# Two expert products replaced by products with the slot matrices in a routed mixture kernel on one Trainium2 core

## The chip, the cores and the metric

The kernel runs on one core of one Trainium2 chip. The metric is the device time of one execution in microseconds (us). The kernel before took 572.39 us, the median of three runs (568.43, 572.39 and 573.89 us).

## The reference, cut to what matters

Three stages follow each other. A decaying linear attention over 4 batches, 8 heads, 768 positions and head size 64 gives 3072 tokens `x` of 512 numbers. A mixture of experts sends each token to one of 8 experts. A second mixture ("slots") forms 32 weighted sums over all tokens, puts each through one of 8 further experts, and hands them back to all tokens.

```
logits = x @ w_gate;  e_idx = argmax(logits);  gate_w = softmax(logits)[e_idx]
eom = sigmoid(x @ w_output_gate)
h = relu(x[mask] @ w1[e])                    # 512 -> 1024, the tokens of expert e
y[mask] = gate_w * eom[mask, e] * (h @ w2[e])        # 1024 -> 512
# the slots, with y as their input
logits = y @ phi                             # 512 -> 32
d = softmax(logits, over the 3072 tokens);  slot_input = d.T @ y     # 32 x 512
slot_out[e] = relu(slot_input[e] @ v1[e]) @ v2[e]    # 4 slots for each of 8 experts
out = softmax(logits, over the 32 slots) @ slot_out
```

## The kernel before, in words

Five programs, one for each engine and one for the DMA queue of SyncE (SP), run in written order and meet at semaphores. There is no planner: the order of the lines is the schedule.

**Attention.** 24 steps of 128 tokens. TensorE (PE) forms scores, outputs and states in plain fp32. Each step also computes the gate logits and stores the finished rows to DRAM. SP loads q, k and v three steps ahead, expert 0's `w1` in between (`load_w1`, in four pieces), and after the last step's loads expert 0's `w2` (`load_w2`).

**Routing.** After the last step VectorE (DVE) finds each token's expert and its rank there. PE multiplies small bf16 matrices (L1256 to L1265) that turn ranks into lists of rows. POOL then gathers the rows of `x` by these lists (`gather_x`).

**Expert chunks.** `for i in range(MAIN)` at L1386 runs 8 chunks, one for each expert, with 432 token places in 4 groups of 108. A chunk does this:
- `x_turn` transposes the gathered rows on PE. ScalarE (`x_high`) and DVE (`x_low`) split the result into two fp32r halves.
- `w1_high`, `w1_low`, `w2_high` and `w2_low` split the weights in the same way, in place, in pieces of 128x1024.
- `h_tile` (8 tiles) and `y_tile` (4 tiles) are the products, 96 fp32r matmuls of 432 columns each per chunk, since `three_pass` multiplies high by high, low by high and high by low. `h_high` and `h_low` keep both halves of `relu(h)`; `y_keep` keeps `y` transposed.
- The slots' share of chunk `i-1` is woven between the h tiles of chunk `i`: `logit_parts` (y times phi, four matmuls side by side in four groups of 32 output partitions), `logits` (the sum of the four parts), `y_turn` (y back to rows), `logits_turn`, `p_turn`, and `acc_part` (p^T times y). On DVE belong to it `logits`, `slot_max`, `max_keep`, `slot_weights` and `accumulate`, on ScalarE `slot_exp`, on POOL `scatter_logits` and `gather_g`. It is a running softmax: `acc` and `ssum` are rescaled by `alpha` in each chunk.

A plain fp32 matmul stands in the trace as two instructions, a transpose or an fp32r matmul as one.

SP loads the next expert's `w1` when all h tiles of a chunk are done (four pieces of 512 KB), then one of the first four `v1` matrices (2 MB), and the next `w2` when all y tiles are done.

**Tail.** `combine_part(MAIN - 1)` does the slots' share of the last chunk by itself. `slot_stage` transposes the slot inputs (L1467), multiplies them with the eight `v1` (L1474), and the result with `v2` in halves (`second_product`), and writes the output in 12 groups (`out_group`). SP loads what is left of `v1` and `v2` there, as buffers come free.

An extra loop for experts with more than 432 tokens exists behind `If(n > MAIN)`; it did not run in this execution.

Of the kernel before, what the change touches and what calls it, by code (L numbers as in the profile page):

```python
# [21 lines left out]
F32 = mybir.dt.float32  # L22
# [3 lines left out]
ALU = mybir.AluOpType  # L26
# [93 lines left out]
def program(nc, qk_h, kv_h, wg_h, phi_h, w1_h, w2_h, v1_h, v2_h, const_h, yscale_h, out_h):  # L120
# [6 lines left out]
    with ExitStack() as ctx:  # L127
# [24 lines left out]
        w2_hi = put("w2_hi", [UNIT], F32R, at=unit(2))  # L152
        w2_raw = put("w2_raw", [UNIT], at=unit(3))
        w2_lo = put("w2_lo", [UNIT], F32R, at=unit(3))
        v_unit = put("v_units", [8, UNIT])
# [16 lines left out]
        acc = put("acc", [P])  # L172
# [8 lines left out]
        hTh = put("hT_hi", [FT, TC], F32R, at=b)  # L181
        hTl = put("hT_lo", [FT, TC], F32R, at=b)
        c_area = b[0]
        yT = put("yT", [KT, TC], at=b)
        yrow = put("y_rows", [NS, D], at=b)
# [8 lines left out]
        a = unit(4)  # L194
# [11 lines left out]
        assert a[0] <= unit(7)[0]  # L206
# [28 lines left out]
        r = [c_area]  # L235
# [9 lines left out]
        r = unit(7)  # L245
        rows = put("rows_hot", [T, SUB], BF16, at=r)
        tcols = put("tile_cols", [T, 3, TW], BF16, at=r)
        assert r[0] <= unit(8)[0]
# [23 lines left out]
        d = [c_area]  # L272
        rs = put("ssum_inv", [1], at=d)
        slotx = put("slot_in", [P], at=d)
# [23 lines left out]
        e = [h_area]  # L298
        v7 = put("v7", [UNIT], at=e)
        hTm = put("hT_masked", [FT, NE, SLOTS], at=e)  # L300
        assert e[0] <= c_area
# [3 lines left out]
        e = [h_area]  # L305
        cT = put("cT", [T, P], F32R, at=e)
        e = unit(3)
# [23 lines left out]
        s_w2 = [sem(f"s_w2_raw{i}") for i in range(NP)]  # L331
# [26 lines left out]
        s_hi1, s_hi2 = sem("s_w1_hi"), sem("s_w2_hi")  # L358
        s_lo1, s_lo2 = sem("s_w1_lo"), sem("s_w2_lo")
# [5 lines left out]
        s_H, s_hh, s_hl = sem("s_h_product"), sem("s_hT_hi"), sem("s_hT_lo")  # L365
        s_Y, s_yT = sem("s_y_product_b"), sem("s_yT")
        s_c1, s_lraw, s_c2, s_lc = sem("s_logit_parts"), sem("s_lraw"), sem("s_logits"), sem("s_lcur")
        s_c3 = sem("s_logits_turned")
        s_yr, s_yk = sem("s_y_turned"), sem("s_y_rows")
# [3 lines left out]
        s_c5, s_acc = sem("s_acc_product"), sem("s_acc")  # L373
# [10 lines left out]
        w1_v = w1_h.rearrange("e (k p) f -> e p k f", p=P)  # L384
        w2_v = w2_h.rearrange("e (k p) m -> e p k m", p=P)
        v1_v = v1_h.rearrange("e (k p) f -> e p k f", p=P)


        V_AT = [v_unit[:, n, :] for n in (4, 5, 6, 7, 0, 1)] + [v6[:, :], v7[:, :]]
        Q_AT = [v_unit[:, n, :].rearrange("p (f h m) -> p h f m", h=2, m=D // 2)[:, half] for half in range(2) for n in (2, 3)]  # L390
        Q_AT += [v_unit[:, n, :].rearrange("p (h f m) -> p h f m", h=2, m=D // 2)[:, half] for n in (4, 5, 6, 7, 0, 1) for half in range(2)]
        OUT_BANKS = ((0, 1), (6, 7))

        OUT = (0, 1, 4)
        Y_BANK = (2, 3, 6, 2)
        X_BANK = (5, 6, 7, 2)
# [29 lines left out]
        def _(sp):  # L426
# [20 lines left out]
            def load_w1(e_, p):  # L447
                sp.dma_start(piece_of(w1_raw, p), w1_v[e_][:, p, :]).then_inc(s_w1[p], 16)

            def load_w2(e_, p):  # L450
                sp.dma_start(piece_of(w2_raw, p), w2_v[e_][:, 2 * p:2 * p + 2, :]).then_inc(s_w2[p], 16)

            def load_v(n):
                sp.dma_start(V_AT[n], v1_v[n]).then_inc(s_v[n], 16)

            def load_v_half(n, half):
                at = slice(half * FF // 2, (half + 1) * FF // 2)
                sp.dma_start(V_AT[n].rearrange("p (k f) -> p k f", f=FF)[:, :, at], v1_v[n][:, :, at]).then_inc(s_v[n], 16)
# [10 lines left out]
            for p in range(NP):  # L469
                load_w2(0, p)  # L470
# [1078 lines left out]
```

## Time and profile before

| what | value |
|---|---|
| median of three runs | 572.39 us |
| the profiled execution: its own time, its span | 566.18 us, 564.3 us |
| PE, DVE, ScalarE (ACT), POOL busy | 92%, 44%, 35%, 24% |
| granted TensorE clock, mean | 0.961 of 2.4 GHz |
| DMA moved | 114.50 MB, mean 203 GB/s |
| the chain that ended last | PE 87%, DMA 5%, DVE 3% |
| L1269 to L1271 (three_pass) in that chain | 55% |

The span runs from the first to the last instruction. An engine's busy share says how long it had something in flight; matmuls overlap in the pipeline, so the duration of one (360 ns for 432 fp32r columns) is nearly twice the distance at which they follow each other. Costs on PE are therefore read from start times.

### The profile page before, as it was taken

The page shows a single profiled execution, that of the slowest core. Times are in us where ns is not written, and L with a number is a line of the kernel's source. Part 1 is how long each engine was busy: PE and PEld are TensorE (multiplying, and loading weights), DVE is VectorE, ACT ScalarE, POOL GpSimd, SP SyncE. Part 2 cuts the span into 40 slices and gives each one's busy share as a digit, 9 for nine tenths or more (in the row PEclk, how much of TensorE's full clock was granted, in tenths as well). Part 3 has the DMA queues.
Part 4 walks back from the last instruction along what each step waited for, and adds up shares of the span by engine and source line. Part 5 has one row for each costly group of instructions (what it writes and reads, how often), then busy time and mean ns, then how long its engine had stood idle before and what let it go on. Part 6 is the DMA issues. An engine that isn't in the chain of part 4 may idle for free.

```text
span 564.3 us, 10969 instructions
## 1 busy us (share of the span) xinstructions
PE 520.6 (92%) x4503; PEld 444.8 (79%) x4503; DVE 250.9 (44%) x425; ACT 195.2 (35%) x370; POOL 136.2 (24%) x143
## 2 busy tenths in 40 slices
PE   6899999925999999999999999999999999969992
PEld 5788788714998999899899899899899989932661
DVE  4565655592443543444363263253354353034332
ACT  2222232301424533444353264262453343120142
POOL 2323323116220250241242143034023023021000
PEclk9999999955999999999999999999999999989996
DMA  8989989704066246428409405406223065988988
GB/s 312 354 319 351 337 326 311 283 20 126 1 218 219 78 162 203 151 98 264 153 25 333 155 4 196 161 8 196 96 76 145 11 204 187 352 305 337 424 315 296
DMA packets 47460, 114.50 MB, mean 203 GB/s; under 512 B 5733, under 2 KB 16894, under 8 KB 45886
## 3 DMA queue, kind: packets, MB, share of 16 engines
q1 hardware_dynamic: 38622, 99.47, 49.6%
q0 software_dynamic: 5200, 7.95, 5.1%
q10 hardware_dynamic: 3600, 6.56, 3.1%
q8 instruction: 27, 0.44, 0.3%
q14 instruction: 11, 0.09, 0.0%
HBM read 100.64 MB, written 13.30 MB: 202 GB/s over the span
## 4 chain that ended last, share of the span: by engine, by line
PE 87%; DMA 5%; DVE 3%; issue 1%; ACT 1%; POOL 0%; SPq 0%; ACTq 0%; POOLq 0%; DVEq 0%
PE bank L1269 19%; PE bank L1270 18%; PE bank L1271 18%; PE bank L1218 4%; PE ybank L1246 4%; PE bank L1474 3%; PE bank L1196 2%; DMA out<-orow 2%; PE bank L1239 2%; PE ybank L1229 2%; PE ybank L1340 2%; PE ybank L1364 1%; PE bank L1193 1%; PE bank L1282 1%; PE bank L1443 1%
## 5 line engine op out<-in xcount | busy, mean ns | idle before, releaser
L1269 PE MATMUL bank<-xT_hi,w_hi 128*128 128x432 f32 x256 | 97.5, 381 | 1.1 <-DVE xT_lo L956 1.1
L1269 PE MATMUL bank<-hT_hi,w_hi 128*128 128x432 f32 x256 | 94.1, 368 | 0.0
L1270 PE MATMUL bank<-xT_lo,w_hi 128*128 128x432 f32 x256 | 92.5, 361 | 0.0
L1271 PE MATMUL bank<-xT_hi,w_lo 128*128 128x432 f32 x256 | 92.2, 360 | 0.0
L1270 PE MATMUL bank<-hT_lo,w_hi 128*128 128x432 f32 x256 | 92.2, 360 | 0.0
L1271 PE MATMUL bank<-hT_hi,w_lo 128*128 128x432 f32 x256 | 91.9, 359 | 0.0
L961 DVE SCALAR_TENSOR_TENSOR hT_lo<-bank,hT_hi 128x432 fp32r<-128x432 f32 x64 | 38.9, 607 | 109.6 <-ACT hT_hi L691 107.9
L570 POOL DMA_INDIRECT slot_logits<-lcur,logit_row_of_row x32 | 32.3, 1008 | 152.7 <-DVE lcur L970 145.4
L691 ACT ACTIVATE hT_hi<-bank 128x432 fp32r<-128x432 f32 x64 | 34.0, 531 | 98.3 <-PE bank L1271 97.9
L1269 PEld LDWEIGHTS bank<-xT_hi,w_hi 128*128 128x128 f32 x256 | 48.6, 190 | 9.7 <-issue 6.3
L695 ACT ACTIVATE yT<-bank 128x432 f32<-128x432 f32 x32 | 17.0, 532 | 107.2 <-PE bank L1271 107.2
L1271 PEld LDWEIGHTS bank<-xT_hi,w_lo 128*128 128x128 f32 x256 | 48.6, 190 | 2.5
L1270 PEld LDWEIGHTS bank<-xT_lo,w_hi 128*128 128x128 f32 x256 | 48.8, 191 | 1.8
L1271 PEld LDWEIGHTS bank<-hT_hi,w_lo 128*128 128x128 f32 x256 | 48.1, 188 | 2.5
L1270 PEld LDWEIGHTS bank<-hT_lo,w_hi 128*128 128x128 f32 x256 | 48.3, 189 | 2.1
L1269 PEld LDWEIGHTS bank<-hT_hi,w_hi 128*128 128x128 f32 x256 | 48.1, 188 | 2.4
L563 POOL DMA_INDIRECT gate_of_row<-gate_scales,token_of_row x32 | 36.0, 1124 | 57.5 <-DVE pT L989 48.5
L557 POOL DMA_INDIRECT xg<-x_rows,token_of_row x32 | 32.2, 1006 | 71.1 <-PE bank L1282 34.0
L826 DVE TENSOR_TENSOR w_lo<-w_raw,w_hi 128x1024 fp32r<-128x1024 f32 x28 | 33.7, 1223 | 21.2 <-ACT w_hi L639 21.2
L830 DVE TENSOR_TENSOR w_lo<-w_raw,w_hi 128x1024 fp32r<-128x1024 f32 x32 | 39.0, 1220 | 8.8 <-ACT w_hi L643 8.8
L838 DVE TENSOR_TENSOR masked_scores<-bank,mask 128x512 f32<-128x512 f32 x48 | 30.9, 686 | 9.3 <-PE bank L1218 9.3
L639 ACT ACTIVATE w_hi<-w_raw 128x1024 fp32r<-128x1024 f32 x32 | 33.1, 1058 | 3.8 <-DMA w_raw<-in_w 3.1
(182 smaller groups left out, 682.3 us busy)
## 6 DMA issues: line engine op xcount, KB each, us to landing
w_raw<-in_w SPq DMA_DIRECT2D x64, 512.0 KB, 6.3
v_units<-in_v SPq DMA_DIRECT2D x20, 1024.0 KB, 11.3
qk<-in_qk SPq DMA_DIRECT2D x24, 512.0 KB, 5.4
kv<-in_kv SPq DMA_DIRECT2D x24, 512.0 KB, 6.2
v_units<-in_v SPq DMA_DIRECT2D x4, 2048.0 KB, 16.4
x_rows<-xrow ACTq DMA_DIRECT2D x25, 256.0 KB, 4.6
out<-orow SPq DMA_DIRECT2D x12, 512.0 KB, 6.0
v<-in_v SPq DMA_DIRECT2D x2, 2048.0 KB, 10.7
```

The costliest lines, as they stand in the source:

```text
L557: pool.indirect_dma_start(xg[0:SUB, s, :], None, x_d, bass.IndirectOffsetOnAxis(ap=at, axis=0)).then_inc(s_xg[s], 16)
L563: pool.indirect_dma_start(gx[0:SUB, s:s + 1], None, g_d, bass.IndirectOffsetOnAxis(ap=at, axis=0)).then_inc(s_gx, 16)
L570: pool.indirect_dma_start(lt_d, bass.IndirectOffsetOnAxis(ap=at, axis=0), lcur[0:SUB, s, 0:SLOTS], None).then_inc(s_ltst, 16)
L639: act.activation(piece_of(w1_hi, p), piece_of(w1_raw, p), ACT.Copy).then_inc(s_hi1, 1)
L691: act.activation(hTh[:, m, :], bank[OUT[m % 3]][:, 0:TC], ACT.Relu).then_inc(s_hh, 1)
L826: dve.tensor_tensor(piece_of(w1_lo, p), piece_of(w1_raw, p), piece_of(w1_hi, p).bitcast(F32), ALU.subtract).then_inc(s_lo1, 1)
L830: dve.tensor_tensor(piece_of(w2_lo, p), piece_of(w2_raw, p), piece_of(w2_hi, p).bitcast(F32), ALU.subtract).then_inc(s_lo2, 1)
L838: dve.tensor_tensor(am[:, 4 * n:4 * n + 4, :], bank[n][:, :].rearrange("p (h t) -> p h t", t=P), mask[:, 4 * n:4 * n + 4, :], ALU.mult).th ...
L961: dve.scalar_tensor_tensor(out=hTl[:, m, :], in0=bank[OUT[m % 3]][:, 0:TC], scalar=0.0, in1=hTh[:, m, :].bitcast(F32), op0=ALU.max, op1=AL ...
L1269: pe.matmul(out, wh, xh, start=first_, stop=False)
L1270: pe.matmul(out, wh, xl, start=False, stop=False)
L1271: return pe.matmul(out, wl, xh, start=False, stop=last_)
```

## The change: what it does

- `y = h w2` is not formed. The slot logits are `h (w2 phi)` and the slot sums are `(p^T h) w2`. `y_tile`, `y_keep`, `y_turn`, `w2_high`, `w2_low`, `h_low` and `acc_part` are gone, and `h` is kept once, in fp32 (`h_keep`).
- `w2 phi` (1024x32 for each expert) is made from a second, transposed copy of `w2` that the host passes in (16 MB more to read): `w2_parts` and `w2_sums`, with copies on ScalarE between them. Experts 0 to 3 are done among the routing's matmuls, ahead of the first `x_turn`; 4 to 7 among the h tiles of chunk 0.
- New in a chunk: `rows_turn` (h back to rows, 32 transposes), `p_times_h`, `product_turn`, `times_w2`, and their copies on ScalarE and DVE; `logit_parts` has 8 matmuls.
- `w1` lies in DRAM by output tiles, so that a piece holds the weights of two h tiles. The next expert's pieces are loaded as pairs of h tiles finish.
- h uses two PSUM banks in place of three. `acc` is 128x512. In the last stage `acc` is transposed, summed and divided by the softmax sum in one product with a scaled summing matrix.

```diff
+            def w2_parts(e_):
+                pe.wait_ge(s_wT[e_], 16)
+                if e_ > 0:
+                    pe.wait_ge(s_wp, e_)
+                for half in range(2):
+                    for k in range(KT):
+                        g_ = slice(k * SLOTS, (k + 1) * SLOTS)
+                        at = k * FF + half * 512
+                        mm = pe.matmul(bank[7 - half][g_, :], phi[:, k, :], WT_AT[e_][:, at:at + 512], start=True, stop=True)
+                mm.then_inc(s_wr, 1)
+            def w2_sums(e_):
+                pe.wait_ge(s_wk, 2 * (e_ + 1))
+                for m in range(FT):
+                    mm = pe.matmul(bank[7][:, m * SLOTS:(m + 1) * SLOTS], ah[:, m * P:(m + 1) * P], slotsum[:, 0:SLOTS], start=True, stop=True)
+                mm.then_inc(s_ws, 1)
...
+            pe.wait_ge(s_lg, T + 2)
+            w2_parts(0)
...
+            w2_sums(0)
+            w2_parts(1)
             pe.wait_ge(s_rpool, 1)
...
             mm.then_inc(s_rp, 1)
+            w2_sums(1)
+            for e_ in range(2, ROUTED):
+                w2_parts(e_)
+                w2_sums(e_)
...
-                out = bank[OUT[m % 3]][:, 0:TC]
+                out = bank[OUT[m % 2]][:, 0:TC]
...
+                for m in range(FT):
+                    g_ = slice(m % 4 * SLOTS, (m % 4 + 1) * SLOTS)
+                    mm = pe.matmul(bank[6][g_, 0:TC], lhs, hT[:, m, :], start=(m < 4), stop=(m >= 4))
...
+            def rows_turn(i, half, s):
+                pe.wait_ge(s_hT, FT * i + 4 * half + 4)
+                for n_ in range(4):
+                    mm = pe.transpose(bank[TURN_BANK[s]][0:SUB, n_ * P:(n_ + 1) * P], hT[:, 4 * half + n_, s * SUB:(s + 1) * SUB], ident)
...
+            def p_times_h(i):
+                for half in range(2):
+                    for s in range(NS):
+                        mm = pe.matmul(bank[2 + half][s * SLOTS:(s + 1) * SLOTS, :], pT[0:SUB, s, :], hrow[0:SUB, s, half * 512:(half + 1) * 512],
+                                       start=True, stop=True)
...
+            def product_turn(i):
+                for half in range(2):
+                    for n_ in range(4):
+                        mm = pe.transpose(bank[7 - half][:, n_ * P:(n_ + 1) * P], ah[:, (4 * half + n_) * P:(4 * half + n_ + 1) * P], ident)
...
+            def times_w2(i):
+                pe.wait_ge(s_ahT, 2 * (i + 1))
+                pe.wait_ge(s_w2, 16 * (i + 1))
+                for m in range(FT):
+                    g_ = slice(m % 4 * SLOTS, (m % 4 + 1) * SLOTS)
+                    mm = pe.matmul(bank[7][g_, :], ahT[:, m, :], w2[:, m * D:(m + 1) * D], start=(m < 4), stop=(m >= 4))
```

PE's order in a chunk is then (`c`: not the first chunk):

```
h0; rows_turn(i-1) 2,3 of half 1; logits(i-1); h1; logits_turn(i-1) or w2_parts(4); h2; w2_sums(4) if not c; h3;
p_turn(i-1) or w2_parts(5); h4; p_times_h(i-1) or w2_sums(5); h5; product_turn(i-1); rows_turn(i) half 0; w2_parts(6) if not c; h6;
w2_sums(6) if not c; x_turn(i+1); h7; times_w2(i-1); logit_parts(i); rows_turn(i) 0,1 of half 1
(in the first chunk after h7: w2_parts(7); two rows_turn; w2_sums(7); logit_parts(0))
```

SP's loads of a chunk, and those before the chunks:

```diff
+            for e_ in range(3):
+                load_wT(e_)
+            sp.wait_ge(s_av, T)
+            load_wT(3)
...
             sp.wait_ge(s_gT, 1)
             sp.dma_start(g_d...).then_inc(s_gst, 16)
+            for s in range(NS):
+                sp.wait_ge(s_xg[s], 16)
+            for e_ in range(ROUTED, NE):
+                if e_ >= 6:
+                    sp.wait_ge(s_wr, e_ - 4)
+                load_wT(e_)
+            for i in range(MAIN):
+                nxt = i + 1 < MAIN
+                if nxt:
+                    sp.wait_ge(s_H, FT * i + 2)
+                    load_w1(i + 1, 0)
+                    sp.wait_ge(s_H, FT * i + 4)
+                    load_w1(i + 1, 1)
+                if i == 0:
+                    sp.wait_ge(s_wr, 1)
+                    load_w2(0)
+                elif nxt:
+                    sp.wait_ge(s_aw, i)
+                    load_w2(i)
+                if nxt:
+                    sp.wait_ge(s_H, FT * i + 6)
+                    load_w1(i + 1, 2)
+                if 1 <= i <= 5:
+                    load_v(i - 1)
+                if nxt:
+                    sp.wait_ge(s_H, FT * i + 8)
+                    load_w1(i + 1, 3)
```

ScalarE and DVE take the new copies in between (`c` as above):

```diff
+                h_keep(i, 0)
+                if c:
+                    rows_keep(i - 1, 1, 2)
+                    w1_high(i, 2)
+                h_keep(i, 1)
+                if c:
+                    slot_exp(i - 1)
+                h_keep(i, 2)
+                if c:
+                    w1_high(i, 3)
+                h_keep(i, 3)
+                h_keep(i, 4)
+                if c:
+                    product_keep(i - 1)
+                if nxt:
+                    w1_high(i + 1, 0)
...
+                if i > 1:
+                    accumulate(i - 2)
+                if c:
+                    rows_keep(i - 1, 1, 1)
+                    logits(i - 1)
+                    rows_keep(i - 1, 1, 3)
+                    w1_low(i, 2)
+                    slot_max(i - 1)
+                    w1_low(i, 3)
+                    max_keep(i - 1)
+                    slot_weights(i - 1)
+                    product_keep(i - 1)
```

## Rows read from the trace of the kernel before

**Rows 1.** The page: span, then busy us, share and instructions of an engine.
```profile
span 564.3 us, 10969 instructions
PE 520.6 (92%) x4503; PEld 444.8 (79%) x4503; DVE 250.9 (44%) x425; ACT 195.2 (35%) x370; POOL 136.2 (24%) x143
```

**Rows 2.** The chain that ended last, in order of time: start us, us, what.
```profile
124.47 0.96 PE ybank L1263 x8
...
135.66 0.97 PE ybank L1282 x4
...
137.88 0.73 PE bank L1269
...
181.59 0.86 PE bank L1321 x8
...
452.27 0.86 PE bank L1321 x8
...
495.69 1.14 PE bank L1328 x8
...
501.94 1.11 PE ybank L1364 x32
...
505.69 16.14 PE bank L1474 x128
```

**Rows 3.** Timeline of PE, chunk 4 and the last y tile: start us, us, engine line op xcount.
```profile
316.57 0.35 PE L1271 MATMUL bank<-xT_hi,w_lo 128*128 128x432 f32 x1
316.86 0.93 PE L1321 MATMUL bank<-yT,phi 128*32 128x432 f32 x8
317.72 0.46 PE L1269 MATMUL bank<-xT_hi,w_hi 128*128 128x432 f32 x1
318.02 0.36 PE L1270 MATMUL bank<-xT_lo,w_hi 128*128 128x432 f32 x1
...
319.98 0.35 PE L1271 MATMUL bank<-xT_hi,w_lo 128*128 128x432 f32 x1
...
323.22 0.36 PE L1271 MATMUL bank<-xT_hi,w_lo 128*128 128x432 f32 x1
...
323.77 0.44 PE L1269 MATMUL bank<-xT_hi,w_hi 128*128 128x432 f32 x1
...
493.13 0.35 PE L1271 MATMUL bank<-hT_hi,w_lo 128*128 128x432 f32 x1
```

**Rows 4.** Timeline of PE's weight loads in the v1 products: start, us, xcount [idle before].
```profile
508.25 0.20 PEld L1474 LDWEIGHTS bank<-v_units,slotT_masked 128*32 128x32 f32 x4 [0.66 <-issue]
...
512.59 0.12 PEld L1474 LDWEIGHTS bank<-v_units,slotT_masked 128*32 128x32 f32 x4 [0.31 <-issue]
```

**Rows 5.** Groups of instructions by line and shape, PE: xcount, busy us, mean ns.
```profile
L1364 PE MATMUL ybank<-y_rows,pT 108*32 108x128 f32 x256 | 8.6, 276 | 0.9 <-ACT y_rows L703 0.9
...
L1432 PE MATMUL bank<-const,c_stack 128*128 128x128 f32 x24 | 3.7, 283 | 0.0
L1479 PE MATMUL ybank<-const,h_raw 128*128 128x32 f32 x16 | 2.0, 277 | 0.7 <-ACT h_raw L789 0.7
```

**Rows 6.** The same view, ScalarE and DVE.
```profile
L691 ACT ACTIVATE hT_hi<-bank 128x432 fp32r<-128x432 f32 x64 | 34.0, 531 | 98.3 <-PE bank L1271 97.9
L703 ACT ACTIVATE y_rows<-ybank 108x512 f32<-108x512 f32 x24 | 14.4, 598 | 5.6 <-PE ybank L1340 5.6
L639 ACT ACTIVATE w_hi<-w_raw 128x1024 fp32r<-128x1024 f32 x32 | 33.1, 1058 | 3.8 <-DMA w_raw<-in_w 3.1 <-issue 0.6
...
L826 DVE TENSOR_TENSOR w_lo<-w_raw,w_hi 128x1024 fp32r<-128x1024 f32 x28 | 33.7, 1223 | 21.2 <-ACT w_hi L639 21.2
L420 DVE COPY orow<-bank 128x512 f32<-128x512 f32 x12 | 8.0, 688 | 6.0 <-DMA out<-orow 3.9 <-PE bank L1461 2.1
```

**Rows 7.** SP's queue: timeline around the routing, then landing of the v_units loads.
```profile
98.67 2.04 SPq L451 DMA_DIRECT2D w_raw<-in_w  x4
...
DMA to landing us min/median/max: 5.0/13.2/25.1
```

**Rows 8.** Stretches: us, busy of each engine, granted clock, DMA share, GB/s.
```profile
110.00:137.90 27.90, 8.91 (x63) 6.37 (x59) 17.19 (x44) 4.60 (x13) 9.15 (x9) 0.57 0.24 70
...
502.00:504.00 2.00, 1.02 (x32) 0.75 (x32) 0.82 (x5) 0.00 (x0) 0.98 (x1) 0.81 1.10 351
...
522.00:540.00 18.00, 17.49 (x237) 10.69 (x238) 5.45 (x9) 2.90 (x13) 0.00 (x0) 1.00 1.01 423
```

More of the change, by code:

```diff
@@ L330, in program @@
         s_w1 = [sem(f"s_w1_raw{i}") for i in range(NP)]
-        s_w2 = [sem(f"s_w2_raw{i}") for i in range(NP)]
+        s_w2 = sem("s_w2")
+        s_wT = [sem(f"s_w2_turned{i}") for i in range(NE)]
+        s_wx = sem("s_w2_phi_extra")
         s_xg = [sem(f"s_x_gathered{i}") for i in range(NS)]
@@ L1389, in _ @@
                 if c:
-                    logit_parts(i - 1)
+                    rows_turn(i - 1, 1, 2)
+                    rows_turn(i - 1, 1, 3)
+                    logits(i - 1)
                 h_tile(i, 1)
                 if c:
-                    logits(i - 1)
+                    logits_turn(i - 1)
+                else:
+                    pe.wait_ge(s_gT, 1)
+                    w2_parts(4)
                 h_tile(i, 2)
-                if c:
-                    y_turn(i - 1, 0)
+                if not c:
+                    w2_sums(4)
@@ L1424, in _ @@
-            n = count_of(pe)
-            combine_part(MAIN - 1)
+                    product_turn(i - 1)
+                for s in range(NS):
+                    rows_turn(i, 0, s)
+                if not c:
+                    w2_parts(6)
+                h_tile(i, 6)
+                if not c:
+                    w2_sums(6)
+                if i + 1 < MAIN:
+                    for s in range(NS):
+                        x_turn(i + 1, s)
+                h_tile(i, 7)
+                if c:
+                    times_w2(i - 1)
+                    logit_parts(i)
+                    rows_turn(i, 1, 0)
+                    rows_turn(i, 1, 1)
+                else:
+                    w2_parts(7)
+                    rows_turn(i, 1, 0)
+                    rows_turn(i, 1, 1)
+                    w2_sums(7)
+                    logit_parts(i)
@@ L1427, in turn_c, with combine_rest @@
+            n = count_of(pe)
+            def combine_rest(i):
+                logits(i)
+                logits_turn(i)
+                p_turn(i)
+                p_times_h(i)
+                product_turn(i)
+                times_w2(i)
+            rows_turn(MAIN - 1, 1, 2)
+            rows_turn(MAIN - 1, 1, 3)
+            combine_rest(MAIN - 1)
             def turn_c(n):
@@ L1514, in _ @@
                             h_tile(i, m)
-                        for m in range(KT):
-                            y_tile(i, m)
-                        combine_part(i)
+                        for half in range(2):
+                            for s in range(NS):
+                                rows_turn(i, half, s)
+                        logit_parts(i)
+                        combine_rest(i)
                 slot_stage()
```

523 lines of the change are left out of this document (243 added, 280 removed).

## The prediction

> **What bounds the kernel now.** I read the page first: PE is busy for 92% of the span, DVE for 44%, ScalarE for 35% [rows 1]. The chain in order of time then gives the stages [rows 2]: routing matmuls end at 125.4, the first h tile starts at 137.9, `logit_parts` comes every (452.27 - 181.59) / 6 = 45.1 us, the v1 products start at 505.7. A `logit_parts` follows the first h tile of its chunk. Taking that tile off (2.4 us, below), chunk 1 starts at 179.2, chunk 0 lasts 41.3 us and chunk 7 starts at 449.9. The reader is to see that a chunk is PE time: in the timeline each matmul starts as the one before lets it. So a chunk shrinks by what PE is spared, until another engine or a load is late. Around the chunks it is otherwise: in 110 to 137.9 PE is busy for 8.9 of 27.9 us at a mean clock of 0.57 of 2.4 GHz [rows 8]; what is added there lies on the path only where DVE or the gathers don't cover it.
>
> **Prices on PE** (distances between starts, not durations, which overlap).
> - fp32r matmul, 432 columns: (319.98 - 318.02) / 10 = 0.197 us [rows 3]. A tile of 12 takes 2.36, the 96 of `y_tile` 18.9.
> - Four transposes between h tiles: 323.77 - 323.22 - 0.197 = 0.35 [rows 3]. Both isolated groups there make the next matmul late by some 0.08 to 0.10 more (318.02 - 317.72 - 0.197 = 0.10), so 0.43.
> - `logit_parts`, 8 instructions: 317.72 - 316.57 - 0.197 + 0.10 = 1.05 [rows 3].
> - fp32, 512 columns, four side by side: four instructions in 0.12 + 0.31 = 0.43 us at full clock, 0.20 + 0.66 = 0.86 at half [rows 4]. So 16 instructions stream in 1.7; at 432 columns eight take 0.72, and 1.05 - 0.72 = 0.3 is the price of going into the group and out. I add it to each group, 2.0 us in all. `p_times_h` contracts over 108 partitions and not 128; `acc_part` did too, and its 32 short instructions took 8.6 / 8 = 1.1 [rows 5], four side by side as well, so I take the same price. Its bounds are 1.7 and, if the four did not overlap, 4 x 1.7 = 6.8.
> - `product_turn`: 8 x 3.7 / 24 = 1.2. `w2_sums` has the form of L1479: 16 instructions, 2.0 [rows 5]. Half a clock doubles each.
>
> The Trainium skill (TensorEngine Tiling (Array Packing), Tiling Modes) says that a change of tiling mode drains TensorE, without a price. The 0.3 us agree with it. Without such a drain the change would have some 16 x 0.3 = 5 us less to pay (one more group in each chunk, and eight `w2_parts`).
>
> **A chunk.** Gone: `y_tile` 18.9, `y_turn` 4 x 0.43 = 1.7, `acc_part` 1.1, `logit_parts` 1.05; 22.8. Added: `rows_turn` 8 x 0.43 = 3.4, `p_times_h` 2.0, `product_turn` 1.2, `times_w2` 2.0, `logit_parts` 1.05 + 0.72 = 1.8; 10.4. A chunk goes from 45.1 to 32.7. Chunks 1 to 6: 6 x -12.4 = **-74.4**.
>
> Is PE still last? ScalarE has 8 x 0.53 for h, 4 x 0.60 for rows, one such for the product, 4 x 1.06 for w1 [rows 6] and some 3.5 for x, parts and exp: 15. DVE has 4 x 1.22 for w1_low, 7 copies or sums from PSUM at 0.69 [rows 6], and some 6 for x_low, logits and the softmax: 16. Both are half of 32.7, so only order can hurt. I walked the orders once: each h tile's bank is freed 1 to 2 us before its turn, and `slot_weights` is done about 1 us before `p_times_h`.
>
> Except for one load. SP waits for `times_w2(i-1)`, near the end of chunk i, before it issues `w2(i)`; w1 piece 2, in chunks 1 to 5 a 2 MB v1 matrix, and w1 piece 3 stand behind that wait in its queue. From 4 us before the next chunk on these are 5.2 MB, at the 423 GB/s of a saturated stretch [rows 8] 12.5 us and some latency, so piece 3 lands 10 to 13 us into the chunk. ScalarE needs it (`w1_high(i, 3)`) between `h_keep` 2 and 3, DVE before `slot_weights`, at 12. I take 1 us for each of five chunks: **+5**. Bounds: nothing; and a landing as late as the slowest v_units load, 25.1 us after issue [rows 7], 10 us in each.
>
> **Routing.** SP issues the last loads before 98.67 [rows 7] and then 3 x 2 MB of turned w2 where 2 MB stood. At 400 GB/s, a little under the 423 shown [rows 8], they land near 110, 115 and 120, the fourth near 126. `w2_parts(0)` starts at 113; it, `w2_sums(0)` and `w2_parts(1)` fit before the routing matmuls, which end at 125.4 as now. After them: sums(1) 2.0 and a copy 0.5; twice parts 1.7, two copies 1.3, sums 2.0; a copy 0.5; `x_turn` 1.6, last `x_high` and `x_low` 1.2. The first h tile starts at 141.1, not 137.9. The gathers, whose last rows PE turned at 135.7 [rows 2], are covered: **+3.2**. [...]
>
> **Chunk 0.** 8 tiles 18.9, four experts' parts and sums 4 x 4.0 = 16.0, `x_turn` 1.6, six `rows_turn` 2.6, `logit_parts` 1.8: 40.9. `w2_parts(4)` comes 4.7 us after the first h tile, but SP loads its data only after `s_gT`, that is, about when that tile starts; 2 MB with a gather beside it take 8 us: 3.5 us of waiting. At the end `w2_sums(7)` waits 1 us for ScalarE, which does four `x_high` first. 45.4 against 41.3: **+4.1**.
>
> **Last chunk and tail.** Now from 449.9 to 564.3: 114.4. After: the chunk up to its last h tile, 32.7 less `x_turn`, `times_w2`, `logit_parts` and two `rows_turn`, 26.5. Then to the v1 products, now 505.7 - 493.3 = 12.4 [rows 2, 3]: `times_w2(6)` and `logit_parts` 3.8, copy and transposes 1.3, the way from `logits` to `pT` 5.8 (501.94 - 495.69 = 6.3 [rows 2], less 0.5 in which `acc_part` waited for rows of y), `p_times_h` 2.0, copy 0.7, turns and sums 2.1, `times_w2` 2.0, accumulate and scale 1.6, slot product and copies 1.8: 21. As PE idles in between, its clock falls (before it fell at 502 to 504 after such a stretch [rows 8]), so 2 more: 23. From the v1 products on the order is the same, 58.6 us; v2's first four halves come 4 us later, which the waits for v1 buffers hide. 108.1: **-6.3**.
>
> **Sum.** -74.4 + 5 + 3.2 + 4.1 - 6.3 = -68.4. The span becomes 495.9; with the 1.9 us around it 497.8, against 566.18 of the profiled execution. That lies 1.1% under the median of the runs (572.39), which would make 503. I predict **499**.
>
> **Rivals.**
> - *The half clock.* The fact for it: 0.57 in the routing and a fall in the tail [rows 8]; against it, PE has work in most gaps. At half clock the matmuls after 125.4 double (9 to 11 us) and `w2_parts(1)` delays routing by 2: 511. 0.12.
> - *Draining of PSUM and row order.* Two banks for h instead of three, ScalarE's queue in strict order: `h_keep` stands behind `slot_exp` and `w1_high`, each of which waits for another. For it: ScalarE already idles 97.9 us for PE's h tiles, none of it needed [rows 6]; against: both engines half idle. Some 2.5 us more in 8 chunks: 519. The Trainium skill (TensorEngine Tiling (Array Packing), Performance Considerations) warns of this very thing, that tiling speeds TensorE but not the copies out of PSUM. 0.13.
> - *Cheaper.* No late piece, no wait in chunk 0, transposes in a row at 0.35: 484. 0.12.
> - *Slower than before.* The late piece 3, alone: each us beyond 12 after chunk start is a us in five chunks. The change loses once those cost 68 us more, 14 each, a landing 27 us into the chunk, 31 after issue. The worst load shown took 25.1 [rows 7]. At 31.5: 575. 0.03.
>
> The forecast has 0.60, for 488 to 510. The range 481 to 519 leaves out the slow rival and the outer ends of two others. A change under 1% could not be told from none here. Faster 0.96, same 0.01, slower 0.03.
>
> **What would show it.** In the trace after: `logit_parts` every 32 to 34 us; first h tile at 141 (at 150 and more: the half clock); PE waiting for a turned w2 after the second h tile of chunk 0; `w1_high` piece 3 waiting for its load in chunks 2 to 6 and `p_times_h` after it; 21 to 24 us between the last h tile and the v1 products. Groups of four at 6.8 in place of 2.0, or PE idle in each chunk over 2 us, would break the sum.

## The result, and the profile after

The changed kernel takes 529.03 us (median of 4 runs, 526.32 to 531.64) against 570.41 of the kernel before beside it (568.2 to 573.89). The ratio is 0.927, 95% interval 0.9195 to 0.9342. The forecast was 499 us in a range of 481 to 519: the direction was right, and so was the place where a chunk would lose time, but the loss there is five times the forecast one, and the time lies 10 us above the range. The profiled execution took 526.32 us, with a span of 524.5 against 564.3 before [rows 1]. The ratios count fast runs alone; among the kernels below only the one of 504.55 us had slow runs, 507.32 and 508.71 us, which stand outside its ratio.

The page of the changed kernel (span, then busy us, share and instructions of an engine), and from its list of costly groups the halves of w1 on ScalarE, to be held against [rows 1] and the third of [rows 6]:

```profile
span 524.5 us, 10518 instructions
...
PE 465.7 (89%) x4254; PEld 350.5 (67%) x4254; DVE 214.1 (41%) x385; ACT 164.1 (31%) x338; POOL 133.8 (26%) x143
...
DMA w_raw<-in_w 19%; PE bank L1340 6%; PE bank L1341 5%; PE bank L1342 5%; PE bank L1264 4%; PE ybank L1292 4%; PE ybank L1427 4%; PE bank L1445 4%; PE bank L1306 3%; PE bank L1312 3%; PE bank L1570 3%; DMA x_rows<-xrow 2%; PE bank L1242 2%; PE bank L1285 2%; PE ybank L1275 2%
...
L665 ACT ACTIVATE w_hi<-w_raw 128x1024 fp32r<-128x1024 f32 x32 | 33.7, 1054 | 51.3 <-DMA w_raw<-in_w 50.6
```

TensorE has 54.9 us less to do, and the time of the profiled executions fell by 39.9. The third line is the chain by line: 19% of the chain that ended last now goes to loads of w1. Before, ScalarE waited 3.1 us for such loads in the whole kernel [rows 6]; now it waits 50.6.

The chain in order of time (start us, us, what), first chunk 0's `logit_parts` (L1382), then one period of the chunk loop and the start of the next, then `logit_parts` of the last chunk and the v1 products (L1570); it answers to [rows 2]:

```profile
196.05 1.59 PE bank L1382 x16
...
229.33 16.04 DMA w_raw<-in_w
245.39 1.07 ACT w_hi L665
246.48 1.22 DVE w_lo L865
248.03 3.54 PE ybank L1427 x16
...
262.99 3.13 PE bank L1445 x16
267.46 16.61 DMA w_raw<-in_w
...
444.07 1.45 PE bank L1382 x16
...
466.35 15.68 PE bank L1570 x128
```

The reader is to see what sets chunks 2 to 6: `times_w2` (L1445), then a load of w1 that takes 16.0 to 17.4 us from issue to use, then ScalarE's and VectorE's halves of it, then `p_times_h` (L1427). These chunks are no longer PE time; they are a loop through SP's queue.

Set against the forecast's span of 495.9, stage by stage (from the start of the first h tile on, cut at the ends of `logit_parts`):

| stage | forecast | measured | difference |
|---|---|---|---|
| first h tile starts | 141.1 | 148.6 | +7.5 |
| chunk 0, to the end of its `logit_parts` | 45.4 | 49.0 | +3.6 |
| chunk 1 | 32.7 | 31.3 | -1.4 |
| chunks 2 to 6 | 5 x 33.7 | 5 x 37.1 | +17.1 |
| last chunk and tail | 108.1 | 110.0 | +1.9 |
| sum | 495.9 | 524.5 | +28.6 |

### The profile page after: what moved, and what is told of

Its sections match the earlier page's. It is cut to its first block, busy times and chain, and to the rows that moved or that the text cites. A ratio compares the mean times of both kernels' runs of the same rounds, so it can differ in the third digit from the quotient of the medians.

```text
span 524.5 us, 10518 instructions
## 1 busy us (share of the span) xinstructions
PE 465.7 (89%) x4254; PEld 350.5 (67%) x4254; DVE 214.1 (41%) x385; ACT 164.1 (31%) x338; POOL 133.8 (26%) x143
## 4 chain that ended last, share of the span: by engine, by line
PE 64%; DMA 23%; ACT 3%; issue 3%; DVE 3%; SPq 2%; POOL 0%; ACTq 0%; POOLq 0%; DVEq 0%
DMA w_raw<-in_w 19%; PE bank L1340 6%; PE bank L1341 5%; PE bank L1342 5%; PE bank L1264 4%; PE ybank L1292 4%; PE ybank L1427 4%; PE bank L1445 4%; PE bank L1306 3%; PE bank L1312 3%; PE bank L1570 3%; DMA x_rows<-xrow 2%; PE bank L1242 2%; PE bank L1285 2%; PE ybank L1275 2%
## 5 line engine op out<-in xcount | busy, mean ns | idle before, releaser
L865 DVE TENSOR_TENSOR w_lo<-w_raw,w_hi 128x1024 fp32r<-128x1024 f32 x28 | 34.3, 1225 | 113.5 <-ACT w_hi L665 109.1
L710 ACT ACTIVATE hT<-bank 128x432 f32<-128x432 f32 x64 | 33.3, 526 | 78.6 <-PE bank L1342 74.7
L597 POOL DMA_INDIRECT slot_logits<-lcur,logit_row_of_row x32 | 32.7, 1021 | 86.2 <-DVE lcur L1014 78.9
L665 ACT ACTIVATE w_hi<-w_raw 128x1024 fp32r<-128x1024 f32 x32 | 33.7, 1054 | 51.3 <-DMA w_raw<-in_w 50.6
L1264 PE MATMUL bank<-qk 64*128 64x128 f32 x384 | 29.7, 297 | 4.0 <-DMA qk<-in_qk 4.0
L1264 PEld LDWEIGHTS bank<-qk 64*128 64x128 f32 x384 | 24.9, 199 | 8.1 <-issue 4.1
L576 POOL TENSOR_TENSOR k_decayed<-kv,const 128x512 f32<-128x512 f32 x20 | 22.2, 1110 | 23.8 <-DMA kv<-in_kv 23.8
L1306 PE MATMUL bank<-units,phi 128*32 128x512 f32 x128 | 21.5, 803 | 5.9 <-issue 4.2
L1427 PE MATMUL ybank<-h_rows,pT 108*32 108x512 f32 x128 | 18.9, 717 | 8.3 <-DVE pT L1033 7.9
L1292 PE MATMUL ybank<-masked_scores,kv 128*64 128x128 f32 x384 | 25.6, 276 | 0.0
L1014 DVE TENSOR_SCALAR lcur<-bank,gate_of_row,pad_mask 108x128 f32<-108x128 f32 x32 | 10.9, 404 | 29.8 <-PE bank L1391 29.8
L573 POOL TENSOR_TENSOR state_decayed<-state,const 128x256 f32<-128x256 f32 x16 | 9.8, 616 | 48.4 <-DVE state L883 33.5
```

What stands on the lines that cost most here:

```text
L597: pool.indirect_dma_start(lt_d, bass.IndirectOffsetOnAxis(ap=at, axis=0), lcur[0:SUB, s, 0:SLOTS], None).then_inc(s_ltst, 16)
L665: act.activation(piece_of(w1_hi, p), piece_of(w1_raw, p), ACT.Copy).then_inc(s_hi1, 1)
L710: act.activation(hT[:, m, :], bank[OUT[m % 2]][:, 0:TC], ACT.Relu).then_inc(s_hT, 1)
L865: dve.tensor_tensor(piece_of(w1_lo, p), piece_of(w1_raw, p), piece_of(w1_hi, p).bitcast(F32), ALU.subtract).then_inc(s_lo1, 1)
L1264: mm = pe.matmul(bank[n][:, a_ * P:(a_ + 1) * P], qk[par][h_, 1, a_, :], qk[par][h_, 0, a_, :], start=True, stop=True)
L1292: mm = pe.matmul(y_at(a_, n), kv[par][:, 1, hd * HD:(hd + 1) * HD], am[:, n * PAIRS + a_, :], start=(c == 0 and a_ < 2), stop=True, skip_g ...
```

## The experiments

Ten kernels ran, in three batches on three chips; beside them the kernel before had medians of 571.95, 570.32 and 570.87 us. Six of the ten ran once. Their totals are set against the profiled execution of the changed kernel (526.32 us), whose four runs alone spread over 5.3 us, so the readings go by stages of the traces. "Period" is the distance between the starts of `logit_parts` of successive chunks.

### Where the chunks lose: three orders of the loads

SP issues four things in a chunk: w2 (behind the wait for `times_w2` of the chunk before), w1 piece 2, a v1 matrix, w1 piece 3. Three kernels have them in another order and nothing else.

First, both w1 pieces ahead of w2:

```diff
                     load_w1(i + 1, 1)
+                if nxt:
+                    sp.wait_ge(s_H, FT * i + 6)
+                    load_w1(i + 1, 2)
+                if nxt:
+                    sp.wait_ge(s_H, FT * i + 8)
+                    load_w1(i + 1, 3)
...
                     sp.wait_ge(s_aw, i)
                     load_w2(i)
-                if nxt:
-                    sp.wait_ge(s_H, FT * i + 6)
-                    load_w1(i + 1, 2)
...
                     load_v(i - 1)
-                if nxt:
-                    sp.wait_ge(s_H, FT * i + 8)
-                    load_w1(i + 1, 3)
```

> In SP's queue the next expert's w1 pieces 2 and 3 go ahead of w2 and v1, so neither stands behind the wait for times_w2. Theory (late pieces: after, chunks 2 to 6 take 37.1 us each and chunk 1, which has no such load, 31.3): the period falls to 31 to 32 us, the waits of ScalarE for w_raw in chunks 2 to 6 (41 us) are gone, and the time falls by 5 x 5.8 = 29 us, to about 498 to 502. Rival (order of the copies out of PSUM, two banks): the pieces arrive but PE still waits for hT and pT; the period stays above 34 and the gain is under 15 us.

Measured: 504.55 us (median of 4, 498.98 to 508.71), ratio 0.875, interval 0.8675 to 0.883. The period is 32.03 us from chunk 2 to chunk 6, as expected. The median lies above the expected 498 to 502: in the profiled execution (507.32 us) the first h tile starts at 157.4, 8.8 us later than in the changed kernel, before any of the loads moved here.

Second, w2 still first, but the v1 matrix behind both pieces (order w2, piece 2, piece 3, v1):

> Only the v1 load moves behind piece 3; w2 and its wait stay ahead of pieces 2 and 3. It tells what the wait costs from what the 2 MB of v1 cost. If transfers are served in order of issue, piece 2 still lands 11 us after issue (as after) and piece 3 comes some 5 us earlier: period about 34.5 to 35.5. If they share the engines, piece 2 comes earlier as well, 7 to 8 us, and the period falls to 32 to 33.

Measured: 517.33 us in one run, mean period 34.7, as expected for transfers served in the order of their issue.

Third, only w2 moved, to the end (order piece 2, v1, piece 3, w2):

> Only w2 and its wait move to the end of the chunk's loads; v1 stays between pieces 2 and 3 and is issued after the sixth h tile. If the wait for times_w2 is the cause, this is as good as putting both pieces first: period 31 to 32 us. If the bytes of v1 ahead of piece 3 matter in themselves, piece 3 is late still and the period is 33 or more.

Measured: 505.2 us in one run, span 503.2, period 32.03.

What ScalarE waits for, from 230 to 415 us (us in total, times, longest us; the two largest waits), in the changed kernel, then with v1 behind the pieces, then with w2 last:

```profile
ACT w_hi L665 <- DMA w_raw<-in_w: 41.1, 10, 7.0
ACT hT L710 <- PE bank L1342: 38.6, 20, 2.4
```

```profile
ACT hT L710 <- PE bank L1342: 49.0, 26, 2.6
ACT w_hi L665 <- DMA w_raw<-in_w: 35.2, 6, 6.4
```

```profile
ACT hT L710 <- PE bank L1342: 78.5, 47, 2.4
ACT p_times_h L722 <- PE ybank L1427: 8.1, 6, 1.4
```

In the changed kernel there are ten waits for w1, two in each of five chunks: one for piece 2, one for piece 3. With v1 out of the way piece 3 is in time and piece 2 stays late; the six waits are about one a chunk. With w2 last there is none, and the v1 matrix ahead of piece 3 does no harm. So w2 with its wait for `times_w2`, standing in front of the pieces, is the cause: 37.1 - 32.0 = 5.1 us a chunk in all. Of these 34.7 - 32.0 = 2.7 come from the late piece 2, and 37.1 - 34.7 = 2.4 from the v1 matrix, which costs only when it stands behind that wait too. What the wait costs and what w2's own 2 MB cost is not told apart by these runs.

How a late piece 2 becomes PE time can be read in one chunk of the changed kernel. SP's timeline (start us, us, engine line op), then ScalarE's and PE's:

```profile
266.14 0.33 SPq L452 DMA_DIRECT2D w<-in_w  x1
266.51 0.43 SPq L449 DMA_DIRECT2D w_raw<-in_w  x1
266.99 0.43 SPq L458 DMA_DIRECT2D units<-in_v  x1
267.46 16.17 SPq L449 DMA_DIRECT2D w_raw<-in_w  x3
```

```profile
270.16 0.60 ACT L718 ACTIVATE h_rows<-ybank 108x512 f32<-108x512 f32 x1
277.75 1.06 ACT L665 ACTIVATE w_hi<-w_raw 128x1024 fp32r<-128x1024 f32 x1 [6.99 <-DMA w_raw<-in_w]
278.71 0.51 ACT L710 ACTIVATE hT<-bank 128x432 f32<-128x432 f32 x1
...
284.10 1.06 ACT L665 ACTIVATE w_hi<-w_raw 128x1024 fp32r<-128x1024 f32 x1 [1.79 <-DMA w_raw<-in_w]
```

w2, piece 2, v1 and piece 3 are issued within 1.3 us (the last line merges piece 3 with the next two loads of w1). Piece 2 (0.5 MB) is used 11.2 us after its issue, piece 3 16.6 us after. While ScalarE stands at piece 2 from 270.76 to 277.75, `h_keep(1)` (the copy of L710 at 278.71) stands behind it in its queue, and PE's h tile 3 wants that bank. Piece 3 holds up `slot_weights` in the same way, and `p_times_h` waits for its pT. All of PE's waits from 230 to 415 us have these two names:

```profile
PE bank L1340 <- ACT hT L710: 9.2, 5, 2.7
PE ybank L1427 <- DVE pT L1033: 7.9, 5, 3.0
```

That is 17.1 us for the five chunks. The periods lose 5 x 5.1 = 25.4. In the remaining 8 us PE was busy longer for the same work, and the granted clock says why: in the four periods in which it averaged 0.95 or 0.96 PE was busy for 33.7 to 34.1 us, in the one at 1.00 (301.7 to 337.7) for 32.4. It is 0.72 in 278 to 284, right after the wait, and 1.00 in a whole period of the kernel with w2 last:

```profile
278.00:284.00 6.00, 4.73 (x18) 4.13 (x19) 2.06 (x4) 2.53 (x6) 0.00 (x0) 0.72 0.81 333
```

```profile
236.00:268.00 32.00, 32.00 (x218) 26.31 (x217) 14.86 (x26) 14.06 (x25) 12.42 (x12) 1.00 0.67 224
```

(columns: stretch, us, busy PE, PEld, DVE, ACT, POOL, granted clock, DMA share, GB/s). The second row also is the forecast's chunk as it was meant: PE busy for all of 32 us, ScalarE for 14, VectorE for 15.

### The routing: turned w2 later, and the half clock

The changed kernel issues the turned w2 of experts 0 to 2 at 100.5, ahead of the last stores of token rows. This kernel issues only the first there, the others after the last attention step's output products:

```diff
-            for e_ in range(3):
-                load_wT(e_)
-            sp.wait_ge(s_av, T)
-            load_wT(3)
+            load_wT(0)
+            sp.wait_ge(s_av, T)
+            for e_ in range(1, ROUTED):
+                load_wT(e_)
```

> Turned w2 of experts 1 and 2 is loaded only after the last attention step, so that 2 MB instead of 6 MB stand beside the last stores of x. Theory (after, the copy into xrow waited 2.7 and 3.2 us for a store and routing began 3.7 us late, with PE at half clock from 116 on): routing starts at 113 again, its list is ready 3.7 to 5 us earlier, and the first h tile starts at 141 to 145 in place of 148.6. Rival: the second expert's data is now late, PE waits for it before the routing matmuls, and nothing is gained.

Measured: 522.99 us in one run. The last gates' products start at 111.47, not 113.87, and the row-number products end 4.6 us earlier, but the first h tile starts at 149.8, 1.1 later than without the edit, where 141 to 145 was expected. PE's timeline shows where it went, first the changed kernel, then this one:

```profile
132.97 1.92 PE L1306 MATMUL bank<-units,phi 128*32 128x512 f32 x16 [0.56 <-ACT w_phi L731]
136.09 1.97 PE L1312 MATMUL bank<-const,p_times_h 128*128 128x32 f32 x16 [1.20 <-ACT p_times_h L726]
138.62 3.36 PE L1306 MATMUL bank<-units,phi 128*32 128x512 f32 x16 [0.56 <-ACT w_phi L731]
```

```profile
129.95 3.64 PE L1306 MATMUL bank<-units,phi 128*32 128x512 f32 x16 [0.56 <-ACT w_phi L731]
134.79 3.62 PE L1312 MATMUL bank<-const,p_times_h 128*128 128x32 f32 x16 [1.19 <-ACT p_times_h L727]
138.97 3.48 PE L1306 MATMUL bank<-units,phi 128*32 128x512 f32 x16 [0.56 <-ACT w_phi L731]
```

`w2_parts` (L1306) takes 1.92 at 2.4 GHz and 3.64 at 1.2, `w2_sums` (L1312) 1.97 and 3.62. The same instructions of PE ran at either clock in the two kernels; why the slower one came with this edit is not shown.

### Chunk 0: two turned matrices ahead of the gates' wait

SP loads the turned w2 of experts 4 and 5 once the x rows are gathered, and waits for the turned gates (`s_gT`) after that:

```diff
-            sp.wait_ge(s_gT, 1)
-            sp.dma_start(g_d..., gT[0:T + 1, :]).then_inc(s_gst, 16)
             for s in range(NS):
                 sp.wait_ge(s_xg[s], 16)
-            for e_ in range(ROUTED, NE):
-                if e_ >= 6:
-                    sp.wait_ge(s_wr, e_ - 4)
+            for e_ in (4, 5):
                 load_wT(e_)
+            sp.wait_ge(s_gT, 1)
+            sp.dma_start(g_d..., gT[0:T + 1, :]).then_inc(s_gst, 16)
+            for e_ in (6, 7):
+                sp.wait_ge(s_wr, e_ - 4)
+                load_wT(e_)
```

> Only the place of two loads on SP's queue changes: the turned w2 of experts 4 and 5 are issued after the first x rows are gathered, ahead of the wait for the turned gates, no longer behind it. Theory (chunk 0 is long because TensorE waits 3.85 us for the turned w2 of expert 4 and then does its partial sums in 3.51 us at half clock): the wait is gone, and chunk 0, from its first h tile to its logit products, takes 44.5 to 46 us and not 49.0; the kernel ends 3 to 4.5 us earlier than after (526.3 in its profile), if its routing ends at the same time. Rival (the wait was hidden under the h tiles that ran at half clock anyway, and what sets chunk 0 is VectorE and ScalarE making the halves of the second chunk's operands): chunk 0 stays within 1 us of 49. The chunks from 2 on stay at 37 us each by both.

Measured: 520.81 us in one run. From the first h tile to the start of `logit_parts` chunk 0 takes 40.7 us, not 47.4; to the end of `logit_parts` 42.4 and not 49.0, where 44.5 to 46 was expected. PE's timeline at `w2_parts(4)`, the changed kernel, then this one:

```profile
159.25 3.51 PE L1306 MATMUL bank<-units,phi 128*32 128x512 f32 x16 [3.85 <-issue]
```

```profile
153.25 1.92 PE L1307 MATMUL bank<-units,phi 128*32 128x512 f32 x16
```

The wait of 3.85 us is gone, and with it 2.8 us more: most of it the partial sums at full clock (1.6) and 0.9 us less of waiting for ScalarE's copy at the end (0.4 for 1.3). 6.6 in all. The whole kernel ends only 5.5 us earlier: the routing gives 1.9, chunks 2 to 6 take 0.7 back, and the last chunk and tail take 2.4. "issue" is the profile's word for a wait it can't name; the edit shows that it was the load.

### The w2-phi work overlapped, and all of it together

With the three edits of order in one kernel (w2 last, turned w2 late, experts 4 and 5 early):

> Three changes of order alone together: w2 last on SP's queue in each chunk, the turned w2 of experts 1 to 3 after the token rows are stored, those of 4 and 5 ahead of the gates. Theory (the costs add): period of a chunk 32.0 as in the run with w2 last (505.2 us), less about 4 for the wait in chunk 0, nothing sure from the routing, since its weights products run at half clock: 499 to 503 us. Rival (the late loads now meet the first chunk's h tiles or w1 in the queues): 505 or above, with a wait for w1 or for a turned w2 in chunk 0.

Measured: 498.51 us in one run, first h tile at 152.2, chunk 0 40.6 us to its `logit_parts`, period 32.03. Against w2 last alone that is 4.8 us less in chunk 0 and 2.9 before it, and 1.1 more in the tail. In this one run the costs add up, as expected.

The next kernel has w2 last, and the chain parts, copies, sums of experts 1 to 3 is opened by giving the odd expert its own banks and buffer:

```diff
+        def parts_at(e_):
+            return (hrow[:, 3, :], 5, 4) if e_ < ROUTED and e_ % 2 else (ah[:, :], 7, 6)
+        def sums_at(e_):
+            return bank[{1: 3, 3: 6}.get(e_, 7)][:, 0:FT * SLOTS]
...
-            w2_sums(1)
             for e_ in range(2, ROUTED):
                 w2_parts(e_)
-                w2_sums(e_)
+                w2_sums(e_ - 1)
+            w2_sums(ROUTED - 1)
```

> w2 last on SP's queue, as in the run of 505.2 us, and in the routing the w2-phi work of experts 1 to 3 is overlapped: the partial sums of the odd expert go to two other PSUM banks and another SBUF buffer, so that TensorE makes the next expert's partial sums while ScalarE copies the ones before, in the order parts 2, sums 1, parts 3, sums 2, sums 3. Theory (the first h tile starts at 148.6 to 155 because parts, copies and sums of experts 1 to 3 stand one behind the other, 18 us from the last rows product): the chain falls by the copies that are now hidden, about 1.4 us each for two experts and their waits, 4 to 6 us, so the first h tile starts 4 to 6 us earlier relative to the product that gives the row numbers, and 499 to 502 us in all. Rival (TensorE's clock is at half there and its products alone fill the stretch, or the gathers of x end it): within 2 us of the run with w2 last, 503.5 to 507.

Measured: 494.17 us in one run, first h tile at 145.8. That is 11 us less than with w2 last alone, where some 4 to 6 were expected; 9.2 of them before the first h tile. The rows are windows from the last row-number product to the first h tile, with w2 last alone, then with the overlap (columns as above):

```profile
131.00:155.00 24.00, 19.45 (x100) 13.27 (x99) 4.50 (x18) 5.59 (x12) 6.29 (x6) 0.57 0.17 43
```

```profile
131.00:145.80 14.80, 13.54 (x106) 10.16 (x106) 5.26 (x22) 5.60 (x12) 6.31 (x6) 0.82 0.26 71
```

PE was idle for 4.6 us of the first and for 1.3 of the second, and the clock was 0.57 and 0.82. 3.3 us of the gain are gaps, the rest is clock. Not all of it is shown to be the edit's: the kernel with w2 last took 23.8 us here, and the changed kernel, with the same order of products, 18.1 at a clock of 0.83. Against that the overlap gains 4.1 us, which is what was expected.

All of them together:

> All of these together: w2 last on SP's queue, turned w2 of experts 1 to 3 after the token rows are stored and of 4 and 5 ahead of the gates, and the overlapped w2-phi work in the routing. Theory (the costs of routing, chunk 0 and late pieces are separate and add up): 505 less 4 (chunk 0), less 4 to 6 (overlap), less 0 to 4 (token rows earlier): 491 to 499 us, first h tile at 140 to 146, period 32.0. Rival (one limit stands behind the others, the half clock of TensorE in the routing, which comes back however the work is ordered): first h tile at 148 or later and 499 to 505 us.

Measured: 490.68 us (median of 6, 487.89 to 493.78), ratio 0.860, interval 0.8556 to 0.8642; first h tile at 143.3, `logit_parts` of chunk 0 at 184.4, period 32.03, all as expected by the first theory, and the time just under its 491 to 499.

### Holding the clock with filler

In the last chunk's chain PE waits for ScalarE and VectorE seven times before the v1 products, 0.4 to 1.8 us each, 7.8 in all. This kernel is the last one with turns of the identity matrix, whose result nobody reads, ahead of those waits:

```diff
+            def fill(n, out):
+                for _ in range(n):
+                    pe.transpose(bank[out][:, 0:P], ident, ident)
...
                 logits(i)
+                fill(12, 0)
                 logits_turn(i)
+                fill(15, 0)
                 p_turn(i)
+                fill(2, 0)
                 p_times_h(i)
+                fill(6, 0)
                 product_turn(i)
+                fill(6, 0)
                 times_w2(i)
+                fill(13, 0)
```

> The best order so far (489.1 us of span, 490.7 us median), and 61 turns of the identity matrix, about 0.11 us each at full clock, are put into the gaps in which TensorE waits in the last chunk's chain (12 before the turned logits, 15 before the turned p, 2, 6 and 6 before p times h, its turn and w2, 13 and 7 before the slot rows). They compute nothing that is used and end before what TensorE waits for, if they run at full clock. Theory (TensorE's clock falls to 0.50 because it waits there, and p times h and w2, 3.64 us each, and the first v1 products run at that half): with the gaps filled the clock stays at 1.00 from 414 to 434 us, p times h and w2 take 1.9 us each, the turn 1.0, and from the last logit products to the first product of the slot sums (41.0 us from 406.4 to 447.4 in the version without filler) it takes 35 to 37. 4 to 6 us less in all: 484.5 to 487. Rival (the clock follows something other than these gaps): the clock stays at half, the fillers themselves take twice as long and delay the chain: 491 to 497.

(Seven more stand before the wait for the masked slot rows.) Measured: 487.15 us (median of 4, 484.61 to 487.81), ratio 0.854, interval 0.8514 to 0.8572, the fastest version here. PE's timeline of that chain, without filler and with it:

```profile
415.58 3.64 PE L1445 MATMUL ybank<-h_rows,pT 108*32 108x512 f32 x16 [0.39 <-DVE pT L1045]
420.03 1.97 PE L1454 MATMUL bank<-const,p_times_h 128*128 128x128 f32 x8 [0.81 <-DVE p_times_h L1012]
422.78 3.64 PE L1463 MATMUL bank<-w,p_times_h_turned 128*32 128x512 f32 x16 [0.78 <-DVE p_times_h_turned L1017]
...
447.37 1.97 PE L1593 MATMUL ybank<-const,h_raw 128*128 128x32 f32 x16 [0.73 <-ACT h_raw L840]
```

```profile
415.39 1.92 PE L1450 MATMUL ybank<-h_rows,pT 108*32 108x512 f32 x16
417.24 0.88 PE L1313 MATMUL bank<-const 128*128 128x128 f32 x6
418.49 1.09 PE L1459 MATMUL bank<-const,p_times_h 128*128 128x128 f32 x8 [0.38 <-DVE p_times_h L1012]
...
420.53 1.92 PE L1468 MATMUL bank<-w,p_times_h_turned 128*32 128x512 f32 x16 [0.29 <-DVE p_times_h_turned L1017]
...
440.76 1.97 PE L1605 MATMUL ybank<-const,h_raw 128*128 128x32 f32 x16 [0.72 <-ACT h_raw L840]
```

And a window of each, columns as above:

```profile
419.00:424.00 5.00, 3.40 (x20) 1.97 (x20) 2.07 (x3) 0.60 (x1) 0.00 (x0) 0.50 0.89 305
```

```profile
419.00:424.00 5.00, 4.71 (x41) 2.82 (x39) 2.66 (x7) 0.00 (x0) 0.00 (x0) 1.00 0.99 402
```

`p_times_h` and `times_w2` take 1.92 in place of 3.64, and the clock stands at 1.00 in place of 0.50. The stretch from the last `logit_parts` (406.3 in both) to the 16 products that read h_raw falls from 41.0 to 34.4 us, with the useful work unchanged. The two kernels with turns in this chain are the only ones in which both products take 1.92; in the nine without, the changed kernel among them, they take 3.3 to 3.6 each, and the stretch 38.8 to 41.1. That settles that the gaps, and not the products, took the clock down there, and that the turns are worth 4.4 to 6.6 us in this stretch. Between the medians only some 3.5 us are seen, and the two intervals of the ratio still overlap.

The same with 26 more turns in the gaps of the routing:

> The version with filler in the last chunk's chain, and 26 more turns of the identity matrix in the gaps of the routing: 10 before the position products, 5, 2 and 2 before the three thirds of the row-number products, 7 before the first h tile. Theory (the half clock in the routing, 0.50 to 0.72 in most stretches from 126 to 150 us, is also paid for with idle TensorE): the first h tile starts 1 to 4 us earlier than the 143.3 us of the version without, and 481 to 486 us in all. Rival (the routing's clock falls for what TensorE does, not for the gaps, since TensorE was busy 5.6 to 6.0 of 6 us at 0.72 there): first h tile at 143 to 147, no gain or a loss of up to 3 us against the filler in the tail alone.

Measured: 487.88 us (median of 4, 484.91 to 490.79), ratio 0.855, interval 0.8496 to 0.8603: no difference to be told from none. The first h tile starts at 141.8, against 142.9 with turns in the tail only and 143.3 without any; 1 us in single executions doesn't decide between the theories. But PE then comes to `w2_parts(4)` 1.3 us before its load, and to one `w2_sums` 1.9 us before ScalarE's copy, and after the second of these gaps the clock is 0.57 from 174 to 180. In that execution more than was won was given back within chunk 0 (45.7 us to its `logit_parts`, against 41.5 in the kernel with filler in the tail only).

## Why the prediction was wrong

**The price of a chunk was right.** With the loads out of the way the period is 32.03, forecast 32.7; chunk 1, which has no late piece, took 31.3. So the balance of 22.8 gone and 10.4 added stands to within 0.7, and so does the price of the new groups: `p_times_h` and `times_w2` take 1.9, forecast 2.0. The rival on draining PSUM (519 us) was close to the time but not its cause: with w2 last PE waits for nothing from 230 to 415. ScalarE's strict order did hurt, but only behind a late load. The Trainium skill (TensorEngine Tiling (Array Packing), Performance Considerations), by which copies out of PSUM could become the limit of tiled products, is not borne out in the chunks here, where ScalarE was busy for 14 of 32 us.

**The step that failed is "except for one load".** It had the right queue and the right wait, listed both w1 pieces behind it, and priced the lateness of one. It said that 5.2 MB stand behind the wait, put piece 3 at 10 to 13 us into the chunk, and took 1 us a chunk. Piece 2 stands behind w2 in the same queue: 2.5 MB, 11.2 us from issue to use. ScalarE wants it before `h_keep(1)`, 7 us earlier than it comes; that alone costs the 2.7 us a chunk that remain with v1 out of the way, and the sum had nothing for it. And piece 3 came 16.6 us after its issue, where 12.5 us and some latency were reckoned; it costs the other 2.4. The rate of 423 GB/s was too high, and other transfers took a share: from 266 to 284 the core moved 6.1 MB and not 5.2, at a mean of 337 GB/s. The first two parts of it:

```profile
266.00:270.00 4.00, 4.00 (x29) 3.60 (x26) 1.72 (x4) 1.40 (x3) 0.00 (x0) 1.00 0.87 261
270.00:278.00 8.00, 6.55 (x42) 5.95 (x39) 1.97 (x5) 1.01 (x3) 3.97 (x4) 1.00 0.98 378
```

The term was +5 and measured 5 x 5.1 = +25.4. It lies inside the bounds that the prediction gave it (nothing to 10 us a chunk), but the range was not stretched to them. Against the forecast, chunks 2 to 6 lose 17.1 us and not 25.4 - 5 = 20.4, since the chunk itself came out 0.7 us cheaper. The signs that the prediction set were met against it: `logit_parts` came every 37.1 us and not every 32 to 34, and PE stood idle for 3.4 us a chunk, over the 2 that would break the sum.

**Routing, +7.5 us.** Every product of this term was priced at the full clock (parts 1.7, sums 2.0), and that failed, as the windows of the changed kernel show, which answer to the first of [rows 8]:

```profile
118.00:130.00 12.00, 10.23 (x64) 5.51 (x56) 10.64 (x21) 3.13 (x8) 1.47 (x1) 0.55 0.72 301
...
138.00:144.00 6.00, 4.25 (x25) 1.56 (x24) 0.00 (x0) 1.47 (x3) 0.00 (x0) 0.72 0.15 49
```

PE was busy for 85% of the first and 71% of the last, and the clock was 0.55 and 0.72. The rival of the half clock (+11 to +13 there, chance 0.12) was the truer one, in part. Of the 7.5 us, 3.6 come before VectorE's first step of the routing, which starts at 116.4 and not at 112.8: ScalarE's `xrow` waits 2.7 and 3.2 us for stores of token rows, 1.84 us of it seen by PE, while 6 MB of turned w2 are on their way. With only 2 MB issued ahead the last gates' products started 2.4 us earlier. Here the prediction counted the DMAs but did not ask what else is in flight. 1.5 come from `w2_parts(1)` at half clock (3.26) ahead of the row-number products, and 2.4 from `w2_parts(3)` (3.36) and the turns of x behind it at half clock.

**Chunk 0, +3.6.** The wait for expert 4's matrix was forecast at 3.5 and measured at 3.85. What was missed is the clock around it: the first ten h products follow each other at 0.36 us and not at 0.197, and the partial sums after the wait take 3.51 us and not 2.0.

**Last chunk and tail, +1.9.** 24.2 us from the last h tile to the v1 products, forecast 23, in which 2 us stood for the clock; from the last `logit_parts` to the products that read h_raw the changed kernel takes 38.8 us, and with the turns 34.4, so the clock costs 4.4 there.

## What to carry over

When a wait is put in front of loads in an in-order queue, list every load behind it with its user and the time it is wanted, and reckon from issue to use by bytes ahead of it; with the load that nobody wants soon at the end the chunks took 25 us less and the kernel some 24 less, more than half of what the whole change had brought. A gap on TensorE cost more than its own length here: 2.8 us beyond the 3.85 at `w2_parts(4)`, 8 beyond the 17.1 in the chunks, 4.4 to 6.6 beyond the 7.8 of the last chunk's chain. So a stage with gaps is to be priced at both clocks, and gaps are worth filling with the next expert's work. An order that brings TensorE early to a later wait can give the gain back.

## What the runs showed of the hardware

- Loads of one queue were served about in the order of their issue. Piece 2 with 2 MB of w2 ahead of it was used 11.2 us after issue, piece 3, with 2 MB of v1 more ahead, 16.6. With v1 behind both, piece 3 was not waited for and piece 2 still was, for up to 6.4 us against 7.0; with w2 behind them no w1 piece was waited for.
- From the last row-number product to the first h tile the same TensorE instructions in the same order took 23.7 to 25.0 us in five kernels (mean granted clock 0.52 to 0.59) and 18.3 and 18.6 in two others (0.83 and 0.82), the changed kernel being one of these. Whether that goes with the kernel or with the single execution is not shown, since each was profiled once; single runs that differ by 6 us there are not to be compared by their sum.
- The identity turns kept the granted clock at 1.00 from 414 to 434 us, where it had been 0.50 or 0.51. The Trainium skill (TensorE: Matmul & The Clock Gate, Part 4: PE-mode transpose) says that transposes don't count as TensorE being busy in the way matmuls do; the trace disagrees, for fp32 turns of 128 x 128 at least. The profile lists them as MATMUL; whether they ran in the transpose mode that the page means is not shown.
